# Expert stage of a fused attention and mixture-of-experts kernel: new order of x and h around the weight split, h turned in its own place

## What is computed

```python
def _moe_ref(x, modality_id, w_gate, modality_bias, w1, w2):
    logits = x @ w_gate + modality_bias[modality_id]
    e_idx = np.argmax(logits, axis=1)
    ...
    for e in range(E):                      # E = 8, D = 512, F = 1024
        mask = e_idx == e
        h = np.maximum(x[mask] @ w1[e], 0.0)
        out[mask] = gate_w[mask, None] * (h @ w2[e])
    return out
```

## Time and profile before

| | us |
|---|---|
| median of 3 runs (1582.21 to 1584.72) | 1582.63 |
| profiled execution, its own time | 1586.44 |
| span of the profiled execution, first to last instruction | 1584.4 |
| PE busy (share of the span) | 1404.6 (89%) |
| DVE busy | 906.9 (57%) |
| ACT busy | 442.9 (28%) |
| POOL busy | 295.8 (19%) |

### The profile page before, as it was taken

How to read it: one execution, slowest core, us unless ns; L and a number is a source line. 1 busy time by engine, 2 the same in 40 slices (tenths; PEclk the granted TensorE clock), 3 DMA queues, 4 the chain that set the end, 5 groups by cost and what they waited for, 6 DMA issues and landing times.

```text
span 1584.4 us, 25118 instructions
## 1 busy us (share of the span) xinstructions
PE 1404.6 (89%) x8270; PEld 1147.7 (72%) x8271; DVE 906.9 (57%) x1509; ACT 442.9 (28%) x766; POOL 295.8 (19%) x364
## 2 busy tenths in 40 slices
PE   5766379979898988986889999999999999999997
PEld 4555367757776777765777888888888888888885
DVE  3557565566646666335677555755565555755551
ACT  4555022222222222223443211421233222422122
POOL 0044323333333343421210000100010000100010
PEclk9788589999999999998999999999999999999999
DMA  9881246466645565445995743274341744234410
GB/s 326 313 309 79 70 143 172 145 180 181 179 130 169 178 183 175 124 109 127 356 330 195 222 149 140 73 194 165 140 166 52 215 150 171 78 127 168 150 68 32
DMA packets 132438, 262.79 MB, mean 166 GB/s; under 512 B 20200, under 2 KB 85736, under 8 KB 126208
## 3 DMA queue, kind: packets, MB, share of 16 engines
q1 hardware_dynamic: 71200, 199.41, 37.9%
q10 hardware_dynamic: 49952, 32.50, 7.9%
q0 software_dynamic: 11200, 29.69, 5.7%
HBM read 179.44 MB, written 51.73 MB: 146 GB/s over the span
## 4 chain that ended last, share of the span: by engine, by line
PE 52%; DVE 14%; issue 12%; DMA 8%; ACT 5%; DVEq 5%; ACTq 2%; SPq 1%; POOL 0%; POOLq 0%
PE ps L1539 28%; PE ps L1519 17%; DVEq L1171 4%; DMA hq<-h 3%; DVE ew L952 2%; DVE ht L1154 2%; DMA mixes<-mix 2%; PE ps L1399 2%; PE ps L1412 2%; DVE xt L1134 2%; ACT hhi L783 2%; ACTq L776 2%; DVE y L1147 1%; PE ps L1509 1%; ACT h L770 1%
## 5 line engine op out<-in xcount | busy, mean ns | idle before, releaser
L1539 PE MATMUL ps<-a_hi,st 128*128 128x512 f32 x1344 | 421.5, 389 | 0.9 <-DVE u L1321 0.9
L1539 PEld LDWEIGHTS ps<-a_hi,st 128*128 128x128 f32 x1344 | 252.3, 188 | 54.4 <-DVE a_lo L1282 1.5
L1519 PE MATMUL ps<-wo,shi 128*128 128x512 f32 x864 | 270.2, 394 | 5.2 <-DVE slo L1291 4.4
L1489 PE MATMUL ps<-ew,hhi 128*128 x640 | 212.0, 414 | 61.3 <-DVE hlo L1161 54.5
L1539 PE MATMUL ps<-a_lo,st 128*128 128x512 f32 x672 | 261.4, 389 | 0.0
L1476 PE MATMUL ps<-ew,xhi 128*128 x640 | 198.7, 392 | 14.8 <-DVE xlo L1139 14.8
L1489 PEld LDWEIGHTS ps<-ew,hhi 128*128 128x128 f32 x640 | 125.0, 199 | 100.5 <-issue 75.3
L1519 PEld LDWEIGHTS ps<-wo,shi 128*128 128x128 f32 x864 | 163.6, 190 | 43.3 <-issue 5.2
L1519 PE MATMUL ps<-wo,slo 128*128 128x512 f32 x432 | 170.9, 396 | 0.0
L665 POOL DMA_INDIRECT out<-ot,out_tok x36 | 36.0, 999 | 720.4 <-ACT ot L829 714.6
L1476 PEld LDWEIGHTS ps<-ew,xhi 128*128 128x128 f32 x640 | 121.1, 189 | 40.2 <-issue 15.0
(11 more groups left out here) (221 smaller groups left out, 1808.5 us busy)
## 6 DMA issues: line engine op xcount, KB each, us to landing
st<-mixes SPq DMA_DIRECT2D x48, 1792.0 KB
raw<-in_moe_w SPq DMA_DIRECT2D x64, 512.0 KB
hq<-h ACTq DMA_DIRECT2D x160, 128.0 KB
mixes<-mix SPq DMA_DIRECT2D x24, 512.0 KB, 8.7
xg<-xs ACTq DMA_DIRECT2D x158, 64.0 KB, 2.7
kt<-in_k SPq DMA_DIRECT2D x8, 1152.0 KB, 10.2
vt<-in_v SPq DMA_DIRECT2D x8, 1152.0 KB, 12.9
qt<-in_q SPq DMA_DIRECT2D x8, 1152.0 KB, 7.9
```

Of the source, the lines that this page charges most:

```text
L1489: last = mm(ps[:, 5 + t.p, :], x[:, rows], weights(e, DC + c // 2, part, cols), start=first, stop=end)
L1519: last = mm(ps[:, 4 + m, :], s[:, rows], wo[f // 2][:, w, f % 2], start=(f == 0 and w == 0 and s is shi[slot]), stop=(f == GC - 1 and s is ...
L1539: last = mm(bank_of(f, idx), st[f % 2][:, at:at + 128], x[:, idx, k, :], start=(k == 0 and w == 0 and x is a_hi), stop=(k == 1 and w == 1))
```

## The change

`xg` becomes a single buffer. `h` and its turned form `ht` no longer share bytes: `ht` is in two halves, the first in a place of its own, the second on the second half of `hlo`. The relu therefore waits for the transfers of the `h` before (`h_in`) instead of for `hlo_made`, and the second half of the turn waits for the `down` of the tile before. ACT's step becomes relu 0 of t, `xhi(t+1)`, relu 1 of t, load of x(t+2), `hhi(t)`. DVE's becomes `split_rest`, `xlo(t+1)`, `split_next`, turn of h(t), `hlo(t)`, turn of x(t+2), y(t-1). PE waits for the split weights two units at a time. The loop ends two tiles earlier and the rest is written out. Before the loop, ACT makes xhi(0) ahead of the load of x(1).

```diff
--- before.py
+++ after.py
@@ -237,15 +237,17 @@
 
 
     expert_place = Place(keep.at)
-    xg = expert_place("xg", [128, 2, 4, 128], F32)
+    xg = expert_place("xg", [128, 4, 128], F32)
     hq = expert_place("hq", [128, 4, F // 4], F32)
     xhi = expert_place("xhi", [128, 2, D], F32R)
     xlo = expert_place("xlo", [128, 2, D], F32R)
-    at_h = expert_place.at
     h = expert_place("h", [128, F], F32)
-    ht = Place(at_h)("ht", [128, FC, 128], F32)
+    ht0 = expert_place("ht0", [128, FC // 2, 128], F32)
     hhi = expert_place("hhi", [128, F], F32R)
+    at_hlo = expert_place.at
     hlo = expert_place("hlo", [128, F], F32R)
+    ht1 = Place(at_hlo + F * 2)("ht1", [128, FC // 2, 128], F32)
+    ht = [ht0, ht1]
     y = expert_place("y", [128, 2, YW], F32)
 
 
@@ -410,10 +412,10 @@
         def tiles(engine, step, after={}):
 
             step(0, 0, False)
-            with engine.Fori(0, (FULL - 2) // 2) as i:
+            with engine.Fori(0, (FULL - 4) // 2) as i:
                 for c in (1, 2):
                     step(i, c, True)
-            for n in range(FULL - 1, NT + 1):
+            for n in range(FULL - 3, NT + 1):
                 step(0, n, True)
                 if n in after:
                     after[n]()
@@ -452,7 +454,7 @@
 
             engine.wait_ge(sorted_in, 32 * t.n + 32)
             for g in quarters:
-                engine.dma_start(xg[32 * g:32 * g + 32, t.p], xs[:, 128 * g:128 * g + 128]).then_inc(x_in[t.p], 16)
+                engine.dma_start(xg[32 * g:32 * g + 32], xs[:, 128 * g:128 * g + 128]).then_inc(x_in[t.p], 16)
 
         @block.sync
         def _(sp):
@@ -754,7 +756,7 @@
                     nc.scalar.copy(yhi0[:, :, cols], yt0[:, :, cols]).then_inc(yhi_made, 1)
 
             def load_x(t, quarters=(0, 1, 2, 3)):
-                wait(act, xt_made, t.n - 1)
+                wait(act, xt_made, t.n)
                 load_quarters(act, t, quarters)
 
             def xhi_of(t):
@@ -762,38 +764,37 @@
                 act.wait_ge(xt_made, t.n + 1)
                 nc.scalar.copy(xhi[:, t.p], xt[:].rearrange("p c t -> p (c t)")).then_inc(xhi_made, 1)
 
-            def h_of(t):
-                for f in range(2):
-                    if f == 0:
-                        wait(act, hlo_made, 2 * t.n)
-                    act.wait_ge(pe_h, 2 * t.n + f + 1)
-                    nc.scalar.activation(h[:, 512 * f:512 * f + 512].rearrange("p (g x i) -> p g x i", g=2, x=FC),
-                                         ps[:, 1 + 2 * t.p + f, :].rearrange("p (g i x) -> p g x i", g=2, x=FC), ACT.Relu).then_inc(h_made, 1)
-                    if f == 0:
-                        wait(act, ht_made, 2 * t.n)
-                    act.wait_ge(h_made, 2 * t.n + f + 1)
-                    for g in (2 * f, 2 * f + 1):
-                        act.dma_start(hq[32 * g:32 * g + 32], h[:, 256 * g:256 * g + 256]).then_inc(h_in, 16)
+            def h_of(t, f):
+                if f == 0:
+                    wait(act, h_in, 64 * t.n)
+                act.wait_ge(pe_h, 2 * t.n + f + 1)
+                nc.scalar.activation(h[:, 512 * f:512 * f + 512].rearrange("p (g x i) -> p g x i", g=2, x=FC),
+                                     ps[:, 1 + 2 * t.p + f, :].rearrange("p (g i x) -> p g x i", g=2, x=FC), ACT.Relu).then_inc(h_made, 1)
+                if f == 0:
+                    wait(act, ht_made, 2 * t.n)
+                act.wait_ge(h_made, 2 * t.n + f + 1)
+                for g in (2 * f, 2 * f + 1):
+                    act.dma_start(hq[32 * g:32 * g + 32], h[:, 256 * g:256 * g + 256]).then_inc(h_in, 16)
 
             def hhi_of(t):
                 for f in range(2):
                     if f == 0:
                         wait(act, pe_y, t.n)
                     act.wait_ge(ht_made, 2 * t.n + f + 1)
-                    nc.scalar.copy(hhi[:, 512 * f:512 * f + 512], ht[:, 4 * f:4 * f + 4, :].rearrange("p x t -> p (x t)")).then_inc(hhi_made, 1)
+                    nc.scalar.copy(hhi[:, 512 * f:512 * f + 512], ht[f][:].rearrange("p x t -> p (x t)")).then_inc(hhi_made, 1)
 
             def tile_step(i, c, has_before):
-                use(Tile(i, c), h_of)
+                use(Tile(i, c), h_of, 0)
+                use(Tile(i, c + 1), xhi_of)
+                use(Tile(i, c), h_of, 1)
                 use(Tile(i, c + 2), load_x)
                 use(Tile(i, c), hhi_of)
-                use(Tile(i, c + 2), xhi_of)
 
             load_x(Tile(0, 0), (0, 1))
-            load_x(Tile(0, 1))
             act.wait_ge(tables_made, 1)
             use = Use(act)
-            for n in range(2):
-                xhi_of(Tile(0, n))
+            xhi_of(Tile(0, 0))
+            load_x(Tile(0, 1))
             tiles(act, tile_step, {FULL - 1: load_first, FULL + 2: y_high})
 
 
@@ -1132,7 +1133,7 @@
                 wait(dve, xhi_made, t.n)
                 wait(dve, xlo_made, t.n)
                 nc.vector.transpose(xt[:].rearrange("p c (t j) -> p t c j", j=32),
-                                    xg[:, t.p].rearrange("p t (c i) -> p t c i", i=32)).then_inc(xt_made, 1)
+                                    xg[:].rearrange("p t (c i) -> p t c i", i=32)).then_inc(xt_made, 1)
 
             def xlo_of(t):
                 dve.wait_ge(xhi_made, t.n + 1)
@@ -1150,15 +1151,18 @@
 
             def h_turned(t):
                 dve.wait_ge(h_in, 64 * (t.n + 1))
+                wait(dve, hlo_made, 2 * t.n)
                 for f in range(2):
-                    nc.vector.transpose(ht[:, 4 * f:4 * f + 4, :].rearrange("p x (t r) -> p t x r", r=32),
+                    if f == 1:
+                        wait(dve, pe_y, t.n)
+                    nc.vector.transpose(ht[f][:].rearrange("p x (t r) -> p t x r", r=32),
                                         hq[:].rearrange("p t (x i) -> p t x i", x=FC)[:, :, 4 * f:4 * f + 4, :]).then_inc(ht_made, 1)
 
             def hlo_of(t):
                 for f in range(2):
                     dve.wait_ge(hhi_made, 2 * t.n + f + 1)
                     cols = slice(512 * f, 512 * f + 512)
-                    nc.vector.tensor_tensor(hlo[:, cols], ht[:, 4 * f:4 * f + 4, :].rearrange("p x t -> p (x t)"), hhi[:, cols].bitcast(F32), ALU.subtract).then_inc(hlo_made, 1)
+                    nc.vector.tensor_tensor(hlo[:, cols], ht[f][:].rearrange("p x t -> p (x t)"), hhi[:, cols].bitcast(F32), ALU.subtract).then_inc(hlo_made, 1)
 
             def split_next(t):
 
@@ -1183,13 +1187,13 @@
                 else:
                     for qn in range(EARLY // 2, UNITS // 2):
                         split(qn)
+                use(Tile(i, c + 1), xlo_of)
                 use(Tile(i, c), split_next)
                 use(Tile(i, c), h_turned)
                 use(Tile(i, c), hlo_of)
+                use(Tile(i, c + 2), x_turned)
                 if has_before:
                     use(Tile(i, c - 1), y_of)
-                use(Tile(i, c + 2), x_turned)
-                use(Tile(i, c + 2), xlo_of)
 
             def y_turned():
                 dve.wait_ge(yin_in, 64)
@@ -1210,7 +1214,6 @@
             gate_values()
             xlo_of(Tile(0, 0))
             x_turned(Tile(0, 1))
-            xlo_of(Tile(0, 1))
             compact_rows()
             tiles(dve, tile_step, {FULL + 1: y_turned, FULL + 3: y_low})
 
@@ -1465,11 +1468,12 @@
             def up(t, e):
 
                 wait(pe, h_made, 2 * (t.n - 1))
-                pe.wait_ge(w_split, UNITS * e + DC)
                 pe.wait_ge(xlo_made, t.n + 1)
                 for f in range(2):
                     cols = slice(512 * f, 512 * f + 512)
                     for c in range(DC):
+                        if f == 0 and c % 2 == 0:
+                            pe.wait_ge(w_split, UNITS * e + c + 2)
                         rows = slice(128 * c, 128 * c + 128)
                         for x, part in ((xhi, 0), (xhi, 1), (xlo, 0)):
                             first, end = c == 0 and x is xhi and part == 0, c == DC - 1 and x is xlo
@@ -1478,9 +1482,9 @@
 
             def down(t, e):
                 wait(pe, y_made[t.p], t.half)
-                pe.wait_ge(w_split, UNITS * e + UNITS)
                 for c in range(FC):
                     if c % 4 == 0:
+                        pe.wait_ge(w_split, UNITS * e + DC + c // 2 + 2)
                         pe.wait_ge(hlo_made, 2 * t.n + c // 4 + 1)
                     rows = slice(128 * c, 128 * c + 128)
                     cols = slice(512 * (c % 2), 512 * (c % 2) + 512)
```

## The result

| | before | after |
|---|---|---|
| median of the runs, us | 1583.7 (1582.2 to 1586.8) | 1568.6 (1565.8 to 1570.4) |
| profiled execution, us | 1586.44 | 1570.40 |
| span, us | 1584.4 | 1568.4 |

The ratio is 0.9901, with a 95% interval of 0.9878 to 0.9923: 15 us faster, where 40 were forecast; 1568.6 lies above the range of 1525 to 1566.

The account below looks back on a forecast made before the run. DVE's queue in split tiles was taken to set most of the 72.5 us over PE's floor. A gain of 57 us, less 17 for the loop of x, left 40 off 1582.6: 1542.6 us, range 1525 to 1566.

Parts of the forecast that it names:

- split tiles: The 25 tiles where DVE also splits two weight units: 13.0 us on average against PE's floor of 10.88.
- the loop of x: Gather, load, landing, next gather through one xs: 10.5 or 12.7 us; long in tiles 7-9 and 21-32, costing 17.
- rival E: Landing of x also takes a second raw load's time: step 13.9, 9 us slower, 1591.7; chance 0.11.
- C: Rival: x long in all 25 split tiles, or control not overlapped: loop 12.5 to 12.8, 18 to 28 off; chance 0.26.
- DVE's own loop: DVE's chain in split tiles, with xlo earlier and y beside control: from 13.0 to 11.65 us on average.
- Relu order: On ACT, xhi between the relus: h lands at 9.0 instead of 11.2; 4.5 us gained in plain tiles, nothing in split tiles.
- plain tiles: The 11 tiles where DVE waits for h, 11.1 to 11.3 us: PE's 10.88 would set them, gaining 0.4 each.
- Single xg: Each load of x waits for the turn of the tile before: cost 0; chain of 9.9 if x is late.
- Start: Before the expert stage's first tiles, xhi(0) no longer stands behind load_x(1) on ACT: 2.2 us gained.
- Tail: After the last tile's up, ACT's y casts come earlier: 8.1 us for 9.5, a gain of 1.4.
- Tile 36: Tile waiting for h behind four y loads on ACT: loss falls from 4.7 to 1.4 us, a gain of 3.3.
- Tile 10: Tile with two splits, waiting for a raw load: loses 1.4 of its 7.2 and uses 1.3 of lead, leaving 4.5.

Follow-up runs that it names:

- run 11: The kernel before, with raw weight loads of experts 1 to 7 cut to 128 of 1024 columns: 1580.7 us, ratio 0.998.
- run 4: The kernel before, with a second xs buffer for the gathered rows: 1579.7 us, ratio 0.997.
- run 7: The kernel before, with only y moved behind the turn of x and ahead of xlo on DVE: 1564.6 us, ratio 0.988.
- run 1: The changed kernel with a second xs buffer for the gathered rows: 1509.2 us, ratio 0.951 to the kernel before.
- Run 6: The changed kernel with two xs, and y put back ahead of the turn of x on DVE: 1507.2 us, ratio 0.951.
- run 15: The kernel before, with y moved behind the turn of x and ahead of xlo, and two xs: 1549.0 us, ratio 0.979.
- run 14: The changed kernel (one xs, one xg), with ACT casting the high part of x ahead of both relus: 1581.1 us, ratio 0.998.
- run 12: The changed kernel with two xs, and ACT casting the high part of x ahead of both relus: 1547.5 us, ratio 0.977.
- run 2: The changed kernel with the second xg buffer given back, one xs as it is: 1571.3 us, ratio 0.990.
- run 5: The changed kernel with two xs and two xg: 1510.5 us, ratio 0.953.
- run 8: The kernel before, with only the new places of xg, h and ht and their waits, old order on ACT and DVE: 1584.0 us, ratio 1.000.
- run 10: The changed kernel with two xs, and PE waiting again for all weights of up and of down at once: 1506.4 us, ratio 0.952.
- run 3: The changed kernel, with raw weight loads of experts 1 to 7 cut to 128 of 1024 columns: 1510.2 us, ratio 0.952.

## Why the prediction was right or wrong

**What bounds the kernel: right.** DVE's queue was last in split tiles. The smaller raw loads and the second xs gave the kernel before 3 and 4 us (runs 11, 4), one swap on DVE gave 19 (run 7).

**The step that failed: the landing in the loop of x.** The prediction named the loop as next and had its gather part right (6.10; the median after is 6.0). The landing was mis-sized. It took 6.64 as the long case, with one raw load in it, and held the short one for "just clear" outside tiles 7-9 and 21-32. After the change the median landing over the 25 split tiles is 7.4, over 6.5 in 20 of them, over 7.5 in 12, and 8.7 at most. Before, the longest was already 7.3, in tile 1, which the prediction's rows do not show. The margin of 0.2 to 0.9 us between the load of x and the raw loads was read off a DVE loop in which x is never late. But once x is late DVE is late, the load waits for its gather (it starts a median 11.25 us after the turn of h, not 6.5), and so it falls on the next raw loads. With small raws, x in time, the load starts at 6.5 as reckoned. Tiles 11 to 13 show it build up: the load starts 6.3, 7.7 and 9.2 after the turn of h and lands in 4.36, 6.48 and 6.87. The lateness sustains itself, and DVE waits for x in 22 of the 25 split tiles. In tiles 7-9 and 21-32 it waits 36.2 us, where 10 to 20 were forecast, and in the others, where none was, 11.7.

Of the mechanisms, rival E's was the right one. In the 11 split tiles in which both raw loads are issued less than 2.65 us after the first issue of the load of x, it lands in 7.6 to 8.7, so the second raw load takes part. Its price was too high: E took 6.64 + 2.28 = 8.92 for the landing and 13.9 for the step. The two tiles shown come to 13.66 (12.29 and 15.03), but only 12 of the 25 landings are over 7.5, and the mean step is 13.05. That is beyond C's 12.5 to 12.8 and short of the 13.5 from which E decides. (C's own terms give 18 to 25 off, not 18 to 28.)

**DVE's own loop: wrong by 0.9, in the other direction.** The forecast was 11.65, and with x in time two tiles in a row take 10.57 and 10.96 (run 1). The prediction let y lie beside control instructions, as it read xlo to do. Run 6 shows that y's place does not matter to the time, and run 15 that y and xlo together in front of the control leave it as long as it was. What counts is that xlo now stands between `split_rest` and `split_next`. Between xlo and the split only the control of the second is left, 1.86. That of the first, 1.8 by the difference to 3.65, now stands ahead of xlo, where in run 1 only 0.40 of idle time is left, put down to ACT's cast. That it runs under DVE's earlier work is read from these rows, and no run isolates it. Run 1, with x nearly always in time, is 16 us under the 1525.6 of the prediction's sum for that case: 25 x 0.4 are the split step (11.23 for 11.65), 4.9 are the start, which the second xs shortens and the sum could not hold, and the rest was not taken apart.

**Relu order: "nothing is gained by it" in split tiles was wrong in its reason.** For h it is right: in split tiles DVE waits for h 0.6 us in all before, 0.8 after and 3.2 in run 14. In plain tiles 4.5 us were forecast for the move through h, and run 14 gives 6.5. But the order also decides when ACT reaches the next load of x. The prediction worked that chain out for the new order, 9.9, and found it under 11.3. It did not work it out for the old one: 5.24 to the load and 6.51 to the next turn are 11.75 (run 12), which is over the 10.57 and 10.96 of run 1. The move is worth 12.5 us in the change (run 14) and 38 with two xs (run 12).

**Single xg: cost 0, right** (runs 2, 5 and 8). The Trainium skill, "Trainium Kernel Development and Optimization", Best Practices, says to double-buffer for performance. By the runs the rule holds for one of the two buffers and not for the other: the second xg is worth nothing and the second xs, the one inside the longest loop, 59 us.

**The small terms.** Plain tiles: a gain of 0.4 each down to 10.88 forecast, some 0.7 measured. Start: 2.2 forecast, 2.6 measured. Tail: 1.4 forecast; 0.6 measured up to the last `down`, 1.6 more in that product itself (5.74 for the 7.38 of the earlier trace rows) and 3.8 after it, which was not taken apart. The 1.6 are the granted clock of TensorE: before, it was 0.57 from 716 to 720 us, mostly the lower of its two levels (1.2 and 2.4 GHz), after a wait of PE of 3.90; after, it was 1.00 throughout that product, after a wait of 3.33. In one execution of each, that is not shown to be the change's doing. Tile 36: 3.3 forecast, 1.2 measured. Tile 10: 1.4 plus lead forecast, 1.2 lost; DVE waits 1.85 for x in that step. Waits for two units, loop bounds and layout: nothing, and nothing measured (runs 10, 8).

## What to carry to other kernels

When a change shortens the queue that is last, the next loop has to be priced with its transfers at the times they will have then, and with every transfer that can overlap it, not with the landings of a trace in which it never was last. Here a loop that was late fell on traffic that it had missed while it was in time, and so stayed late. And a cast or relu in front of a load in an engine's queue is part of that load's loop: write that loop out for the old order as well as for the new, for each buffer and for the queue itself.

## What the runs showed of the hardware

The landing of x, 256 KB from one on-chip place to another in four parts, depends on when the nearest raw loads of 512 KB are issued, though by another engine. Counted from the first issue of the load of x:

| load of x | raw loads issued | landed |
|---|---|---|
| before, 507.27 | 2.75 and 4.8 later | 4.36 |
| before, 494.53 | 2.03 and 4.3 later | 6.64 |
| after, 496.51 | 0.73 and 2.8 later | 6.78 |
| after, 482.64 | 0.59 ahead, 1.67 later | 7.95 |
| after, 509.38 | 0.15 and 2.2 later | 7.96 |

Between the first two rows 0.7 us of distance make 2.3 us of landing, and the step between them is sharp. In the kernel before, 24 of the 25 split tiles have raw loads beside the load of x. In the 14 in which the first raw load was issued 2.18 us or more after the first issue of x, x landed in 4.33 to 4.53. In the 10 in which it was 2.17 or less, it took 6.42 to 7.31. The four issues of x take 2.52 us in all, so the boundary lies within the issue of the fourth part, as the prediction had read it. It is not the whole of it: in the changed kernel a load with its first raw load 2.29 later, in tile 1, took 6.85. That is how thin the margin was that the prediction called clear. With the raw loads cut to an eighth, all 25 landings of run 11 and 23 of the 25 of run 3 were under 5. The Trainium skill, "DMA: Bandwidth & Descriptors", section "Issuing engines are not separate DMA queues", says that transfers started by different engines run on the same DMA engines and interleave. The trace agrees: raw loads issued by SP make a load issued by ACT 2.3 us longer.

What DVE's branches and register loads cost depends on where they stand. With those of `split_rest` and `split_next` together behind xlo, 3.97 us pass between xlo and the split (mean of 25 tiles before). With xlo between the two, 1.90 pass behind it (run 1), and the idle time ahead of xlo is 0.40 in the tile shown. A second short operation back to back in front of both made them no shorter (4.09 in run 15).
